# Filter spectra for four steps in one burst, units for two steps at once, and one PSUM bank for the way back, in a long convolution ahead of two feed-forward layers

## The reference

```python
def _attn_ref(x, v, pos_emb, w1, w2):          # x, v: 1 x 12480 x 128, pos_emb: 12480 x 64
    h_mlp = np.maximum(pos_emb @ w1, 0.0) @ w2
    h_filt = h_mlp * np.exp(-0.01 * np.arange(S))[:, None]
    u, L = x * v, 2 * S
    Uf, Hf = np.fft.rfft(u, n=L, axis=1), np.fft.rfft(h_filt, n=L, axis=0)
    y = np.fft.irfft(Uf * Hf[None, :, :], n=L, axis=1)[:, :S, :]
    return x * y
# then two feed-forward layers on the 12480 x 128 result:
#   relu(x @ w_in)**2 @ w_out,   and   (max(h, 0) + alpha * min(h, 0)) @ w_out2,   d_ff = 2048
```

## Time and profile before

| what | value |
|---|---|
| median of three runs | 1385.48 us (1385.04 to 1386.36) |
| the profiled execution | 1383.66 us, span 1381.8 us |
| PE, PE weight loads | 1368.9 us busy (99%), 1155.9 us (84%) |
| DVE, ACT, POOL | 1118.5 us (81%), 1122.3 us (81%), 180.0 us (13%) |
| DMA | 75.35 MB, mean 55 GB/s |

### The profile page before, as it was taken

The page is one execution under the profiler, slowest core; times in us unless marked ns, Lnnn a source line. Parts: engine busy times, 40 slices in busy tenths (PEclk is TensorE's granted clock), DMA queues, the critical chain, the costliest instruction groups (busy, mean ns, idle before and its releaser), DMA issues.

```text
span 1381.8 us, 19839 instructions
## 1 busy us (share of the span) xinstructions
PE 1368.9 (99%) x6879; PEld 1155.9 (84%) x6879; DVE 1118.5 (81%) x1399; ACT 1122.3 (81%) x1504; POOL 180.0 (13%) x202
## 2 busy tenths in 40 slices
PE   9999999899999999999999999999999999999998
PEld 8988888898888888888888888888888888888887
DVE  6888889468778878887888788887888878888888
ACT  3778888258778877887888888888888888888887
POOL 4547888410000000000000000000000000000000
PEclk9999999999999999999999999999999999999999
DMA  8538897520010110000000000000000000000000
GB/s 268 176 118 255 275 284 222 171 90 1 28 32 1 31 32 13 27 0 9 8 8 8 0 9 8 8 0 8 9 8 8 0 8 9 8 8 0 9 9 15
DMA packets 53587, 75.35 MB, mean 55 GB/s; under 512 B 5357, under 2 KB 37587, under 8 KB 53507
## 3 DMA queue, kind: packets, MB, share of 16 engines
q1 hardware_dynamic: 46995, 64.24, 14.8%
q10 hardware_dynamic: 6384, 9.99, 2.4%
q0 software_dynamic: 128, 0.02, 0.0%
HBM read 54.93 MB, written 19.23 MB: 54 GB/s over the span
## 4 chain that ended last, share of the span: by engine, by line
PE 94%; DVE 2%; ACT 2%; DMA 1%; issue 1%; SPq 0%; POOL 0%; ACTq 0%; DVEq 0%
PE ps L188 13%; PE ps L190 13%; PE ps L189 13%; PE ps L203 12%; PE ps L205 12%; PE ps L204 12%; PE ps L758 5%; PE ps L795 3%; PE ps L874 3%; PE ps L773 3%; PE ps L781 2%; PE ps L766 1%; PE ps L741 1%; DVE stage L398 1%; PE ps L842 1%
## 5 line engine op out<-in xcount | busy, mean ns | idle before, releaser
L412 DVE TENSOR_TENSOR g_lo<-stage,g_hi 128x1024 fp32r<-128x1024 f32 (+2 forms) x199 | 238.2, 1197 | 165.3 <-ACT g_hi L313 164.7
L188 PE MATMUL ps<-x_hi,w_hi 128*128 128x512 f32 (+2 forms) x800 | 310.7, 388 | 0.5 <-DVE x_lo L382 0.3
L203 PE MATMUL ps<-g_hi,w_hi 128*128 128x512 f32 (+2 forms) x800 | 309.1, 386 | 2.0 <-DVE g_lo L444 1.4
L190 PE MATMUL ps<-x_lo,w_hi 128*128 128x512 f32 (+2 forms) x800 | 307.7, 385 | 0.0
L189 PE MATMUL ps<-x_hi,w_lo 128*128 128x512 f32 (+2 forms) x800 | 307.6, 385 | 0.0
L205 PE MATMUL ps<-g_lo,w_hi 128*128 128x512 f32 (+2 forms) x800 | 307.5, 384 | 0.0
L204 PE MATMUL ps<-g_hi,w_lo 128*128 128x512 f32 (+2 forms) x800 | 307.4, 384 | 0.0
L322 ACT ACTIVATE relu<-ps 128x1024 f32<-128x1024 f32 (+2 forms) x200 | 201.6, 1008 | 111.2 <-PE ps L190 108.4
L398 DVE SCALAR_TENSOR_TENSOR stage<-stage,alpha_sb 128x512 f32<-128x512 f32 (+2 forms) x400 | 276.2, 732 | 0.4 <-ACT stage L355 0.2
L355 ACT ACTIVATE stage<-ps,sign_sb 128x512 f32<-128x512 f32 (+2 forms) x400 | 250.9, 672 | 2.3 <-PE ps L190 1.0
L444 DVE TENSOR_TENSOR g_lo<-g,g_hi 128x1024 fp32r<-128x1024 f32 (+2 forms) x200 | 239.0, 1195 | 12.9 <-ACT g_hi L343 12.8
(11 more groups left out here) (68 smaller groups left out, 1217.8 us busy)
## 6 DMA issues: line engine op xcount, KB each, us to landing
g_dram<-work SPq DMA_DIRECT2D x49, 256.0 KB, 3.5
work<-dft_back SPq DMA_DIRECT2D x66, 128.0 KB, 3.2
gt<-g_dram SPq DMA_DIRECT2D x10, 784.0 KB
gt<-x_seq SPq DMA_DIRECT2D x32, 196.0 KB
work<-v_seq SPq DMA_DIRECT2D x32, 196.0 KB
work<-dft_forward SPq DMA_DIRECT2D x49, 128.0 KB, 3.4
x<-x_gate ACTq DMA_DIRECT2D x16, 390.0 KB, 4.6
out_t<-x SPq DMA_DIRECT2D x23, 256.0 KB, 2.0
```

The costliest lines, as they stand in the source:

```text
L188: nc.tensor.matmul(into[:, c, :t], w_hi[k][:, at], x_hi[layer][:, :t], start=True, stop=False)
L190: last = nc.tensor.matmul(into[:, c, :t], w_hi[k][:, at], x_lo[layer][:, :t], start=False, stop=True)
L203: nc.tensor.matmul(acc[layer][:, :t], w_hi[k][:, at], hi[:, c], start=first, stop=False)
L412: nc.vector.tensor_tensor(lo[:, :, :t], g2[at][:, :, :t], hi[:, :, :t].bitcast(FP32), ALU.subtract).then_inc(g2_lo_ready, 1)
```

## The change

The units are now computed and copied for two steps at once, in odd iterations: (k+4, k+5) in iteration k, into the whole of bank 2, and ACT's copy puts them back over the rows of `a_r` that they came from, so that `r_hat` needs no buffers. The filter spectra use four banks, 4 to 7, and are computed for four steps at once in every fourth iteration (two steps each in iterations 0 and 2). All ways back use bank 3. ACT does the result copy first in every iteration. The forward tables get seven slots. The banks of the six early inverse passes after the loop are renumbered.

```diff
--- before.py
+++ after.py
@@ -510,9 +510,9 @@
     pos_sb = a_u[:, :HID * R]
 
     taken[0] = shared
-    FW, INV = 5, 4
-    forward, back = carve(FW, 2, P), carve(INV, 2, P)
-    r_hat = [w.rearrange("p (r k) -> p r k", r=2) for w in (w1_and_window, carve(2 * P))]
+    FW, INV = 7, 4
+    forward = carve(FW, 2, P)
+    back = [w.rearrange("p (r k) -> p r k", r=2) for w in (w1_and_window, *(carve(2 * P) for _ in range(INV - 1)))]
     filt = carve(2, 2, 4 * P)
     assert taken[0] <= shared + HID * P
     SUMS = 3
@@ -537,13 +537,33 @@
     def short_steps(k):
         return k - sum(map(is_long, range(k)))
 
-    def unit_bank(k):
-        return 6 if k == 0 else 2 + k % 2
+    def r_hat(k):
+
+        return a_r_rows[:, 2 * k:2 * k + 2]
+
+    def unit_columns(steps):
+
+        return ps[:, 6 if 0 in steps else 2, :2 * P * len(steps)]
+
+    def units_in(k):
+
+        first = 3 if k == 0 else k + 4
+        return range(first, first + 2) if (k == 0 or k % 2) and first < K_STEPS else range(0)
+
+    def filters_in(k):
+
+
+        return range(k + 1, k + 1 + {0: 2, 2: 2}.get(k, 4 if k % 4 == 0 else 0)) if k + 1 < K_STEPS else []
 
     def filter_banks(k):
 
 
-        return ps[:, 6:8, :2 * P] if k == 0 else ps[:, 4:6, 2 * P * ((k - 1) % 2):2 * P * ((k - 1) % 2 + 1)]
+        if k == 0:
+            return ps[:, 6:8, :2 * P]
+        pair, half = divmod((k - 1) % 4, 2)
+        return ps[:, 4 + 2 * pair:6 + 2 * pair, 2 * P * half:2 * P * (half + 1)]
+
+    INVERSE_BANK = 3
 
     def two_banks(b):
         return ps[:, 2 * b:2 * b + 2, :].rearrange("p b w -> p (b w)")
...
@@ -759,13 +779,17 @@
                                         dft98_sb[:], start=True, stop=True)
             last.then_inc(spec_done, 1)
 
-        def unit_spectra(k):
-            pe.wait_ge(forward_loaded[k % FW], 16 * (k // FW + 1))
-            wait(pe, r_hat_copied, k - 1)
-            for i in range(2):
-                last = nc.tensor.matmul(ps[:, unit_bank(k), P * i:P * (i + 1)], a_r_rows[:, 2 * k + i],
-                                        forward[:, k % FW, i], start=True, stop=True)
-            last.then_inc(r_hat_done, 1)
+        def unit_spectra(steps):
+            if not steps:
+                return
+            wait(pe, r_hat_copied, steps[0])
+            for n, k in enumerate(steps):
+                pe.wait_ge(forward_loaded[k % FW], 16 * (k // FW + 1))
+                for i in range(2):
+                    at = P * (2 * n + i)
+                    last = nc.tensor.matmul(unit_columns(steps)[:, at:at + P], a_r_rows[:, 2 * k + i],
+                                            forward[:, k % FW, i], start=True, stop=True)
+                last.then_inc(r_hat_done, 1)
 
         def u_spectra(k):
             wait(pe, u_used, k - 1)
@@ -776,9 +800,11 @@
 
         def filter_spectra(k):
             pe.wait_ge(r_hat_copied, k + 1)
+            if k % 2:
+                pe.wait_ge(filt_copied, max(1, k - 2))
             for i in range(2):
                 for blk in range(NB):
-                    last = nc.tensor.matmul(filter_banks(k)[:, blk, P * i:P * (i + 1)], r_hat[k % 2][HALF[blk], i],
+                    last = nc.tensor.matmul(filter_banks(k)[:, blk, P * i:P * (i + 1)], r_hat(k)[HALF[blk], i],
                                             w2_sb[HALF[blk], P * blk:P * (blk + 1)], start=True, stop=True,
                                             tile_position=(N1 * blk, 0))
             last.then_inc(filt_done, 1)
@@ -787,12 +813,12 @@
             pe.wait_ge(y_ready, k + 1)
             for n in tables(k):
                 pe.wait_ge(back_loaded[n % INV], 16 * (n // INV + 1))
-            wait(pe, g_copied, k - 1)
+            wait(pe, g_copied, k)
             for i in range(2):
-                out, at = ps[:, 6 + k % 2, 256 * i:256 * (i + 1)], slice(256 * i, 256 * (i + 1))
+                out, at = ps[:, INVERSE_BANK, 256 * i:256 * (i + 1)], slice(256 * i, 256 * (i + 1))
                 data = (sums[:, k % SUMS, at], crossed[:, at])
                 for n, y in zip(tables(k), data):
-                    last = nc.tensor.matmul(out, back[:, n % INV, i], y, start=n == tables(k)[0], stop=n == tables(k)[-1])
+                    last = nc.tensor.matmul(out, back[n % INV][:, i], y, start=n == tables(k)[0], stop=n == tables(k)[-1])
             last.then_inc(inv_done, 1)
 
         warm_up()
@@ -804,14 +830,13 @@
             if n == EARLY_UNITS:
                 pe.wait_ge(copied_0, units_end)
                 pe.wait_ge(copied_1, units_end)
-                unit_spectra(0)
+                unit_spectra(range(1))
             if n == EARLY_FILTER:
                 pe.wait_ge(w2_loaded, 16)
                 filter_spectra(0)
         pe.wait_ge(copied_0, len(chunks) - 1)
         pe.wait_ge(copied_1, len(chunks) - 1)
-        unit_spectra(1)
-        unit_spectra(2)
+        unit_spectra(range(1, 3))
         for k in range(K_STEPS + 2):
             if k == 0:
                 pe.wait_ge(copied_0, len(chunks))
@@ -820,20 +845,17 @@
                 u_spectra(k)
             for h in {K_STEPS: (0, 1), K_STEPS + 1: (2,)}.get(k, ()):
                 first_pass(pe, h)
-            if k + 3 < K_STEPS:
-                unit_spectra(k + 3)
+            unit_spectra(units_in(k))
             if k >= 2:
                 inverse(k - 2)
-            if k % 2 == 0 and k + 2 < K_STEPS:
-                wait(pe, filt_copied, k + 1)
-                filter_spectra(k + 1)
-                filter_spectra(k + 2)
+            for n in filters_in(k):
+                filter_spectra(n)
         for h in (3, 5, 4):
             first_pass(pe, h)
 
     def half_bank(h):
 
-        return 2 + h if h < 2 * EARLY_GROUPS else 6 + h % 2
+        return (2, 4, 5, 6, INVERSE_BANK, 7)[h] if h < 2 * EARLY_GROUPS else 6 + h % 2
 
     def half_pass(h, half):
 
@@ -850,10 +872,10 @@
             pe.wait_ge(idft98_loaded, 16)
         if h % 2 == 0:
             pe.wait_ge(half_0_loaded[h // 2], 16)
-        if half_bank(h) >= 4:
+        if half_bank(h) == INVERSE_BANK:
+            pe.wait_ge(g_copied, K_STEPS)
+        elif half_bank(h) > 2:
             pe.wait_ge(filt_copied, K_STEPS)
-        if half_bank(h) >= 6:
-            pe.wait_ge(g_copied, K_STEPS - half_bank(h) % 2)
         half_pass(h, 0).then_inc(first_passed, 1)
 
     def sum_half(pe, h):
@@ -895,11 +917,12 @@
         return src.rearrange("p c k -> p k c"), out[HALF[part], :, blk, CH * j:CH * (j + 1)]
 
     def scalar_program(act):
-        def unit_copy(k):
-            act.wait_ge(r_hat_done, k + 1)
-            wait(act, filt_done, k - 1)
-            nc.scalar.copy(r_hat[k % 2].rearrange("p r k -> p (r k)"), ps[:, unit_bank(k), :2 * P]
-                           ).then_inc(r_hat_copied, 1)
+        def unit_copy(steps):
+            if not steps:
+                return
+            act.wait_ge(r_hat_done, steps[-1] + 1)
+            rows = a_r_rows[:, 2 * steps[0]:2 * steps[-1] + 2]
+            nc.scalar.copy(rows.rearrange("p r k -> p (r k)"), unit_columns(steps)).then_inc(r_hat_copied, len(steps))
 
         def filter_copy(k):
             act.wait_ge(filt_done, k + 1 + k % 2)
@@ -920,7 +943,7 @@
         def result_copy(k):
             act.wait_ge(inv_done, k + 1)
             wait(act, g_stored[k % 3], 16 * (k // 3))
-            nc.scalar.copy(g_sb[:, k % 3].rearrange("p r w -> p (r w)"), ps[:, 6 + k % 2, :]).then_inc(g_copied, 1)
+            nc.scalar.copy(g_sb[:, k % 3].rearrange("p r w -> p (r w)"), ps[:, INVERSE_BANK, :]).then_inc(g_copied, 1)
             if k >= K_STEPS - DIRECT:
                 act.wait_ge(g_copied, k + 1)
                 for q in range(k + 1 + DIRECT - K_STEPS):
@@ -963,22 +986,18 @@
                 last = nc.scalar.copy(dst, src)
             last.then_inc(copied_0, 1)
             if n == EARLY_UNITS:
-                unit_copy(0)
+                unit_copy(range(1))
             if n == EARLY_FILTER:
                 filter_copy(0)
-        unit_copy(1)
-        unit_copy(2)
+        unit_copy(range(1, 3))
         pieces = {**{18 + n: n for n in range(4)}, **{28 + n: 4 + n for n in range(4)},
                   **{43 + n: 8 + n for n in range(4)}}
         for k in range(K_STEPS + 2):
-            if k % 2 == 0 and k >= 2:
+            if k >= 2:
                 result_copy(k - 2)
             if k + 1 < K_STEPS:
                 filter_copy(k + 1)
-            if k % 2 and k >= 2:
-                result_copy(k - 2)
-            if k + 3 < K_STEPS:
-                unit_copy(k + 3)
+            unit_copy(units_in(k))
             if 2 <= k - 3 < 2 + RAWS:
                 load_raw(k - 5)
             for n in range(GATES):
```

More of the change, by code:

```diff
@@ L640, in load_back @@
         def load_back(n):
-            sp.dma_start(back[:, n % INV], ap["dft_back"][n]).then_inc(back_loaded[n % INV], 16)
+            sp.dma_start(back[n % INV], ap["dft_back"][n]).then_inc(back_loaded[n % INV], 16)
         step = HID // POS * R
```

## The result

| | before | changed |
|---|---|---|
| median | 1385.26 us (1383.81 to 1386.36, 4 runs) | 1394.27 us (1393.27 to 1394.73, 4 runs) |
| ratio | | 1.0063, 95% interval 1.0051 to 1.0074 |
| span of the profiled run | 1381.8 us | 1392.6 us |

What follows compares the result with a forecast made beforehand. PE was taken as only just bounding the loop, with DVE close behind. Start +1.9, steps 8 to 44 +5.6, rounding copies +1.7 and loop's end +0.7 gave +9.9 us: forecast 1395 us, range 1386 to 1400.

Steps and rivals of the forecast that it cites:

- The walk of twelve steps: Steps 8 to 20 of the loop, each start the latest of what it waits for: 40.34 us against 38.30.
- What bounds the loop: In the frequency loop PE is only just the bound; DVE has little left, 35.2 of 38.30 us in twelve steps.
- Fewer bursts: Filter bursts in the loop fall from 24 to 13, each saving 0.40 us of array-shape change: 4.4 us less PE stream.
- One bank: In the loop, way back k-2 must wait for result copy k-3; not priced singly, only within the walk.
- The second rival: Only the bank costs: 0.09 us a turn, 24 times, and some 1.5 at the start; 1384.8 us, chance 0.09.
- Result copy first: In odd steps ACT's filter copy waits for the way back, delaying DVE, then PE; not priced singly.
- Unit pairs, seven tables: Odd steps' ways back come 0.45 us later, even ones' 0.45 earlier; tables cost nothing, bounds 1.7 us either way.
- Start: Steps 0 to 8: units 5 and 6 wait for the copy of units 3 and 4; +1.9 us.
- Rounding copies: Four of ACT's twelve rounding copies (steps 18, 19, 29, 30) fall where ACT is late: +1.7 us.
- Loop's end: Step 44 to the last way back takes 19.7 us against 19.33, plus 0.3 for rounding copies: +0.7 us.
- The third rival: New waits in the loop drop the clock to half rate for 10 to 20 us: 1400 to 1405 us, chance 0.04.
- What would show it: Loop signs: 12 or 13 burst idles, result copies awaited, odd filter copies 0.7 us late, DVE's filter-copy waits 20 us or more.

Runs made afterwards that it cites:

- the first experiment: The changed kernel, but in odd iterations ACT does the filter copy before the result copy again, as in the kernel before: 1398.87 us, ratio 1.0093.

## Why the prediction was right

Forecast were 1395 us, slower with 0.82; measured 1394.27. Step by step:

- *The walk of twelve steps.* Forecast 40.34 us, measured 40.28 in the first period and 40.27, 40.26 and 40.27 with the rounding copies moved. In detail, relative to u(8) at 113.06, u(10) stands at 7.63 (7.63), u(11) at 9.83 (9.90), u(14) at 21.03 (21.05), u(15) at 23.76 (23.73). Four others, which start with an unhidden weight load of 0.11 that the walk counts before the start, are with it at 5.02 (5.00), 13.76 (13.75), 18.42 (18.42) and 27.16 (27.17). DVE agrees as well: its steps 10, 14 and 18 start at 10.17 (10.17), 23.57 (23.59) and 37.84 (37.89), after waits of 1.19, 0.67 and 1.54 us, where the walk lost 0.98, 0.6 and 1.5.
- *What bounds the loop.* The prediction called PE "only just the bound". It did not name the ring through PE, ACT, DVE and POOL that the traces show, but its walk followed that ring's waits one by one, and for that reason came out right where a sum over PE would not have.
- *Fewer bursts, 4.4 us less in PE's stream.* Right as a size, and none of it reached the time. The prediction gave the longer bursts no price; at this place of the units they cost 5.2 us against bursts of two.
- *One bank.* The forecast gave it no price of its own. It is 18.8 us alone, in ACT's old order. The new order takes back 4.6 between two kernels with pairs and long bursts, and pairs and long bursts together 5.0 in the old order; the parts don't add up singly. The second rival, which gave it 0.09 us a turn, was wrong at the point named against it: ACT isn't free when a way back ends. The forecast took this rival for the time of one bank without ACT's new order (1384.8); that order left as it was, the bank alone gave 1403.89.
- *Result copy first.* The link step by step is in the trace. Its price alone is 2.8 us.
- *Unit pairs, seven tables.* Nothing that shows (ratio 0.9985 to 1.0005), as costed for the tables. The place of the pairs was worth more than anything else in PE's order: 7.7 us.
- *Start.* +1.9 forecast, +1.82 measured. The cause named for it, the wait of units 5 and 6, carries 0.7. Of the other 1.1, 0.45 is DVE's later step 1, behind the later first burst; the remainder I haven't traced.
- *Rounding copies.* +1.7 forecast, 1.75 measured.
- *Loop's end.* +0.7 forecast, +0.39 measured.
- *The third rival.* Its mechanism exists, as the first experiment shows, behind waits of 2.00 and 1.89 us, longer than any of PE's in the changed kernel's loop (1.42).
- *Sum.* The loop was forecast at +9.9 and grew by 9.3. The 1.3 us behind it, the clock's longer stay at its lower level in a stretch where it falls in both kernels, were not forecast; the profiled run was 10.7 us above that of before, the medians 9.0. That the medians come out so close to 1395 has some luck in it.
- *What would show it.* PE's weight loads before bursts idle 13 times, result copies are waited for, and the filter copy starts 0.69 us behind the slot (0.7 forecast). Of the ways back 12, 16 and 17 that the walk let wait for the one bank, 12 and 16 do in the first period (weight loads at 134.99 and 149.25, the result copies' ends at 134.87 and 149.14), 17 doesn't. One sign was badly named: DVE's waits put down to filter copies fell from 11.1 to 8.9 us instead of growing to 20, because 12.0 us of DVE's standing still are listed under "issue", where no one releaser is shown. All idle time before DVE's first instructions of a step grew from 17.5 us (15.9 + 1.6) to 26.4 (19.1 + 7.3).

## What to carry to other kernels

Before time is taken out of the busiest engine's stream, ask what the freed resource was bought with: here 4.4 us of PE time were paid with the second output bank, and that bank alone was worth 18.8 us in the kernel before because its reader, ACT, is a queue that serves others first. When several engines pass work round in a ring with less than a microsecond of slack, walk one full period, here twelve steps, with durations and signal delays from the trace; it came within 0.2% of the period, where the work of PE alone sums to 36.2 us and that of DVE to 35.2. And put work that nobody waits for behind work that heads a queue elsewhere.

## What the runs showed of the hardware

- Changing from full-array to half-height products and back cost 0.40 us per burst in every kernel (the idle 0.33 us before the first weight load is the same for bursts of 16, 24 and 32 records). The change costs by the number of bursts, not by their length.
- An ACT copy of 128x512 from PSUM lets the next instruction start after 0.48 us and is seen by others after 0.59. The walk needed both numbers.
- In the kernel with ACT's old order a wait of 2.00 us inside the loop was followed by the lower clock level, with the way back at 3.36 us instead of 1.97; another wait of 2.00 us in the same loop, ended at 200.18, was not (1.00 from 200 to 204), though PE had been busy for about as long before it (3.17 of 5 us, against 3.00). So such a wait can cost more than its length, and not each time.
- After the same idle of 3.9 us behind the loop, the granted clock stayed at its lower level long enough to make the same 32 product records 1.3 us longer in one kernel than in the other. Spans of single runs differ by that without a change in the work.
